# Fused attention and two feed-forward layers on one Trainium2 core: queries and keys split by pairs of heads on GpSimd and placed by DMA copies in SBUF

## The reference

```python
scores = (q @ k.T) / sqrt(D)
cum = cumsum(max(s, 0))
bias = -(cum[:, None] - cum[None, :])
scores = where(causal, -1e9, scores + minimum(bias, 0))
attn = softmax(scores)
x = attn @ v                      # then heads side by side: (2304, 512)
h = x @ w_in; solu = h * softmax(h); x = layernorm(solu) * g_ln @ w_out
out = maximum(x @ w1, x @ w2, x @ w3) @ w_out2
```

## Time and profile before

| what | value |
|---|---|
| median of 3 runs | 772.84 us (771.74 to 778.02) |
| the profiled execution's own time | 775.42 us |
| its span, first to last instruction | 773.3 us |
| mean granted TensorE clock | 0.993 |
| PE busy | 727.6 us (94%) |
| DVE busy | 418.7 us (54%) |
| ACT busy | 328.3 us (42%) |
| POOL busy | 225.7 us (29%) |

### The profile page before, as it was taken

The page is one execution under the profiler, slowest core; times in us unless marked ns, Lnnn a source line. Parts: engine busy times, 40 slices in busy tenths (PEclk is TensorE's granted clock), DMA queues, the critical chain, the costliest instruction groups (busy, mean ns, idle before and its releaser), DMA issues.

```text
span 773.3 us, 12787 instructions
## 1 busy us (share of the span) xinstructions
PE 727.6 (94%) x4312; PEld 662.6 (86%) x4312; DVE 418.7 (54%) x766; ACT 328.3 (42%) x795; POOL 225.7 (29%) x240
## 2 busy tenths in 40 slices
PE   3898999899899899999999999999999999999997
PEld 2777788788787788989898989999989999899995
DVE  8999999999985675535444364513203123032120
ACT  2888888888784443423233243412112121121111
POOL 6756669878762631404040200000000000000000
PEclk9999999999999999999999999999999999999999
DMA  6465464545341110106100031000010000100101
GB/s 154 115 165 139 135 149 119 131 124 143 88 91 43 42 37 6 41 1 176 29 0 0 0 109 56 1 21 22 1 42 1 14 28 0 41 0 0 41 0 42
DMA packets 46580, 45.28 MB, mean 59 GB/s; under 512 B 22164, under 2 KB 37652, under 8 KB 46516
## 3 DMA queue, kind: packets, MB, share of 16 engines
q1 hardware_dynamic: 46548, 44.86, 22.2%
HBM read 39.43 MB, written 5.38 MB: 58 GB/s over the span
## 4 chain that ended last, share of the span: by engine, by line
PE 66%; DMA 8%; POOL 7%; DVE 6%; issue 6%; SPq 4%; ACT 2%; POOLq 0%; ACTq 0%
PE ps L600 10%; PE ps L602 10%; PE ps L601 10%; DMA qk_raw<-in_qk_dram 8%; PE ps L532 4%; PE ps L534 4%; PE ps L533 4%; PE ps L520 4%; PE ps L522 4%; PE ps L521 4%; PE ps L613 3%; PE ps L614 3%; PE ps L615 3%; POOL qk_b L671 2%; POOL v_hl L675 2%
## 5 line engine op out<-in xcount | busy, mean ns | idle before, releaser
L602 PE MATMUL ps<-x_lo,w_hi 128*128 (+1 forms) x432 | 144.4, 334 | 0.0
L600 PE MATMUL ps<-x_hi,w_hi 128*128 128x384 f32 x432 | 144.3, 334 | 0.0
L601 PE MATMUL ps<-x_hi,w_lo 128*128 128x384 f32 x432 | 144.3, 334 | 0.0
L783 ACT ACTIVATE probs<-ps,nmax 128x576 f32<-128x576 f32 (+4 forms) x160 | 82.7, 532 | 14.2 <-DVE nmax L1002 14.2
L793 ACT ACTIVATE pt_hi<-ps 128x512 fp32r<-128x512 f32 (+1 forms) x128 | 69.7, 570 | 35.3 <-PE ps L432 32.6
L414 PE MATMUL ps<-k_a,q_a 128*128 128x288 f32 (+2 forms) x192 | 70.0, 369 | 12.9 <-DVE q_a L995 12.3
L432 PE MATMUL ps<-ident,probs 128*128 128x128 f32 x480 | 74.6, 285 | 7.7 <-DVE pt_lo L1009 3.1
L600 PEld LDWEIGHTS ps<-x_hi,w_hi 128*128 128x128 f32 x432 | 81.1, 188 | 0.2
L601 PEld LDWEIGHTS ps<-x_hi,w_lo 128*128 128x128 f32 x432 | 81.1, 188 | 0.2
L602 PEld LDWEIGHTS ps<-x_lo,w_hi 128*128 128x128 f32 x432 | 81.1, 188 | 0.0
L1009 DVE TENSOR_TENSOR pt_lo<-ps,pt_hi 128x512 fp32r<-128x512 f32 (+1 forms) x128 | 77.9, 649 | 3.4 <-ACT pt_hi L793 2.2
(11 more groups left out here) (102 smaller groups left out, 1469.1 us busy)
## 6 DMA issues: line engine op xcount, KB each, us to landing
qk_raw<-in_qk_dram SPq DMA_DIRECT2D x64, 288.0 KB, 4.3
rinvB<-rsum_dram SPq DMA_DIRECT2D x24, 192.0 KB, 4.0
stage<-in_moe_w_dram SPq DMA_DIRECT2D x18, 256.0 KB, 4.2
out_dram<-stage SPq DMA_DIRECT2D x18, 256.0 KB, 2.0
v_raw<-in_v_dram SPq DMA_DIRECT2D x32, 128.0 KB, 2.4
stage<-in_moe_w_out_dram SPq DMA_DIRECT2D x14, 256.0 KB, 2.7
stage<-in_moe_w_in_dram SPq DMA_DIRECT2D x4, 512.0 KB, 3.3
aux_dram<-setup SPq DMA_DIRECT2D x1, 576.0 KB, 4.6
```

Of the source, the lines that this page charges most:

```text
L600: pe.matmul(dst, w_hi[f][:, i, c, :], x2_hi[par][:, c, :], start=(c == 0), stop=False)
L601: pe.matmul(dst, w_lo[f][:, i, c, :], x2_hi[par][:, c, :], start=False, stop=False)
L602: mm = pe.matmul(dst, w_hi[f][:, i, c, :], x2_lo[:, c, bass.ds(g * GT, GT)], start=False, stop=(c == KC - 1))
L783: act.activation(dst, SCORES[c], ACT.Exp, bias=nmax[par][:, c:c + 1], accum_out=sums_all[:, c, bass.ds(t, 1)]).then_inc(exp_done, 1)
```

## The change

1. **Load by pairs.** A new layout `qk` holds a pair of heads on 128 partitions, k first. One DMA of 128x2x576 per pair (L286 of the changed kernel) replaces four of 64x1152. It lands in `split`, which for each of two pair buffers has four rows per partition: 0 high k, 1 high q, 2 raw k (then low k), 3 raw q (then low q).
2. **Split on GpSimd.** `scale_q` scales the raw q in place, `qk_high` writes both high parts with one instruction, `qk_low` overwrites the raw parts with the low ones. For head pair 0 these are shared out over GpSimd, ScalarE and VectorE. VectorE's `q_low` is gone from the slots; ScalarE's `split_v` goes to GpSimd too.
3. **Place by DMA.** TensorE's operands live in `oper`, one for each parity: rows `k_a`, `q_a`, `q_b`, `k_b`. Three DMAs from SBUF to SBUF per head (`copy_high`, and two in `copy_low`, each 64x2x576, 288 KB) put the halves in their places, after the head before last has its scores; the aux load follows. TensorE waits for `oper_loaded` (3 copies and aux) in place of four semaphores.
4. **First chunk on 64 partitions.** `first_of(c)` replaces the padding: chunk 0 is rows 0 to 63. The matmuls of chunk 0 have 64 stationary columns, the transposes of block column 0 have 64, `pt_high` and `pt_low` of group 0 take 448 columns instead of 512 and those of group 1 64 partitions instead of 128; `q_b` x `k_b` uses 68 partitions of 128. The memsets of the padding go.
5. **A moved wait.** TensorE waits for all of `pt_lo` of the slot before ahead of the chunk 0 scores and no longer in `turn(1)`.

```diff
+            def load_qk(pair, pb):
+                sp.dma_start(split[:, pb, 2:4, :], qkT[bass.ds(pair, 1)].rearrange("a p i s -> (a p) i s")).then_inc(qk_loaded[pb], 16)
...
+            def copy_high(h, pb):
+                rows = slice(D * h, D * (h + 1))
+                sp.dma_start(f32(oper[h][0:D, 0:2, :]), split[rows, pb, 0:2, :]).then_inc(oper_loaded[h], 16)
+
+            def copy_low(h, pb):
+                rows = slice(D * h, D * (h + 1))
+                sp.dma_start(f32(oper[h][D:P, 0:2, :]), split[rows, pb, 0:4:3, :]).then_inc(oper_loaded[h], 16)
+                sp.dma_start(f32(oper[h][0:D, 2:4, :]), split[rows, pb, 1:3, :]).then_inc(oper_loaded[h], 16)
...
             load_qk(0, 0)
+            load_qk(1, 1)
             load_v(0, 0)
-            load_qk(1, 1)
-            sp.wait_ge(rows_zeroed, 2)
+            load_v(1, 1)
+            sp.wait_ge(k0_hi_ready, 1)
+            sp.wait_ge(q0_hi_ready, 1)
+            copy_high(0, 0)
+            sp.wait_ge(k0_lo_ready, 1)
+            sp.wait_ge(q0_lo_ready, 1)
+            copy_low(0, 0)
             sp.wait_ge(cum_ready, 1)
             for h in range(2):
...
+                sp.dma_start(f32(oper[h][D:D + 4, 2:4, :]), rows).then_inc(oper_loaded[h], 16)
+            copy_high(1, 0)
+            copy_low(1, 0)
             sp.dma_start(aux_dram, setup[:, :, :]).then_inc(aux_stored, 16)
...
+            def reload_qk(pair, pb):
+                sp.wait_ge(oper_loaded[0], pair * 64 - 64)
+                sp.wait_ge(oper_loaded[1], pair * 64 - 64)
+                load_qk(pair, pb)
+
+            def refill(pair, h, pb):
+                t = 2 * pair + h
+                if h == 0:
+                    sp.wait_ge(lo_ready, pair)
+                    sp.sem_inc(sp_passed, 1)
+                sp.wait_ge(scores_done, 3 * (t - 1))
+                copy_high(h, pb)
+                copy_low(h, pb)
+                load_aux(t, h)
...
+            def reload_pair(pair, pb, known=None):
+                if known is None or known + 2 < PAIRS:
+                    reload_qk(pair + 2, pb)
+                if known == 0:
+                    sp.wait_ge(aux_stored, 16)
+                refill(pair + 1, 0, 1 - pb)
+                if known != 0:
+                    reload_v(2 * pair + 1, 1)
+                refill(pair + 1, 1, 1 - pb)
+                reload_v(2 * pair + 2, 0)
...
             def scores_4(t, par, known):
-                pe.wait_ge(q_hi_ready, t + 1)
-                pe.wait_ge(k_hi_ready, t + 1)
-                pe.wait_ge(q_lo_ready, t + 1)
-                pe.wait_ge(k_lo_ready, t + 1)
-                pe.wait_ge(aux_loaded[par], (t - par) * 8 + 16)
+                pe.wait_ge(oper_loaded[par], (t - par) * 32 + 64)
...
                     score_pass(SCORES[3], 0, 4 * P - PAD, 3, par, 3 * P - PAD)
+                    if live(known, 1) and known != 1:
+                        pe.wait_ge(pt_lo_done, 4 * (t - 1))
                     score_pass(SCORES[0], 0, P - PAD, 0, par, 0).then_inc(scores_done, 1)
...
+            def scale_q(pair, pb):
+                pool.wait_ge(qk_loaded[pb], (pair - pb) * 8 + 16)
+                q = split[:, pb, 3, :]
+                pool.tensor_scalar(q, q, SCALE, 1.0, ALU.mult, ALU.mult).then_inc(q_scaled, 1)
+
+            def qk_high(pair, pb):
+                pool.wait_ge(q_scaled, pair)
+                pool.tensor_scalar(split[:, pb, 0:2, :].bitcast(F32R), split[:, pb, 2:4, :], 1.0, 1.0, ALU.mult,
+                                   ALU.mult).then_inc(hi_ready, 1)
+
+            def qk_low(pair, pb):
+                pool.wait_ge(hi_ready, pair)
+                raw = split[:, pb, 2:4, :]
+                pool.tensor_tensor(raw.bitcast(F32R), raw, split[:, pb, 0:2, :], ALU.subtract).then_inc(lo_ready, 1)
...
+            def slot(pair, half_, pb, known):
+                t = 2 * pair + half_
                 if live(known, 1):
+                    split_v(t - 1, 1 - half_, None if known is None else known - 1)
+                if live(known, -4 + half_):
+                    if half_ == 0:
+                        scale_q(pair + 2, pb)
+                        qk_high(pair + 2, pb)
+                    else:
+                        qk_low(pair + 2, pb)
...
             def slot(t, par, known):
-                if live(known, -1):
-                    q_low(t + 1, 1 - par)
                 if live(known, 0):
```

More of the change, by code:

```diff
@@ L18, with first_of @@
 MASKED = -1.0e9
+def first_of(c):
+    return 0 if c == 0 else P * c - P // 2
 def chunk_offset(c):
-    return P * c * (c + 1) // 2
+    return sum(first_of(i + 1) for i in range(c))
 def attention_and_mlp(nc, qkT, v, s, w_in, w_out, g_ln, w1, w2, w3, w_out2, out):
-    HEADS, D, _, S = qkT.shape
+    PAIRS, _, _, S = qkT.shape
+    HEADS, D = 2 * PAIRS, P // 2
     DM, FF = w_in.shape
@@ L120, in attention_and_mlp @@
             setup = sb(a, "setup", [HEADS, 8, S])
-            qk_raw = [sb(a, f"qk_raw{i}", [P, 2, S]) for i in range(2)]
+            split_t = sb(a, "split", [P, 2, 4, ROW])
             v_raw = [sb(a, f"v_raw{i}", [P, NCH, D]) for i in range(2)]
@@ L126, in attention_and_mlp @@
             vlo_b = sb(a, "vlo_b", [D, QB])
-            q_a = [sb(a, f"q_a{i}", [P, SP], F32R) for i in range(2)]
-            qk_b = [sb(a, f"qk_b{i}", [P, SP + S], F32R) for i in range(2)]
-            k_a = [sb(a, f"k_a{i}", [P, S], F32R) for i in range(2)]
+            oper_t = [sb(a, f"oper{i}", [P, 4, ROW], F32R) for i in range(2)]
             ident_b = sb(a, "ident_b", [P, P], BF16)
@@ L136, in attention_and_mlp @@
             pt_lo = [sb(a, f"pt_lo{i}", [P, TW], F32R) for i in range(2)]
-        q_raw, k_raw = [t[:, 0, :] for t in qk_raw], [t[:, 1, :] for t in qk_raw]
-        q_b, k_b = [t[:, 0:SP] for t in qk_b], [t[:, SP:SP + S] for t in qk_b]
+        split, oper = split_t[:, :, :, 0:S], [t[:, :, 0:S] for t in oper_t]
+        k_a, q_a, q_b, k_b = [[t[:, i, :] for t in oper] for i in range(4)]
         one_rows = [setup[:, i, :] for i in (0, 2, 5, 7)]
@@ L284, in _ @@
             sp.dma_start(s_sb, s).then_inc(s_loaded, 16)
-            def load_qk(h, par):
-                rows = qkT[bass.ds(h, 1)].rearrange("a d i s -> (a d) (i s)")
-                for copy in range(2):
-                    dst = qk_raw[par][D * copy:D * (copy + 1), :, :].rearrange("p i s -> p (i s)")
-                    sp.dma_start(dst, rows).then_inc(qk_loaded[par], 16)
+            def load_qk(pair, pb):
+                sp.dma_start(split[:, pb, 2:4, :], qkT[bass.ds(pair, 1)].rearrange("a p i s -> (a p) i s")).then_inc(qk_loaded[pb], 16)
@@ new lines, in _ @@
+            reload_pair(0, 0, 0)
+            reload_pair(1, 1, 1)
+            with sp.Fori(1, 1 + KC // 2) as quad:
+                for i in range(2):
+                    pair = 2 * quad + i
+                    reload_pair(pair, i)
+                    sp.dma_start(stage[:, bass.ds(pair * FF - 2 * FF, FF)], w_in[bass.ds(pair * P - 2 * P, P), :]).then_inc(w_loaded, 16)
+            with sp.Fori(1 + KC // 2, 1 + KC // 2 + FB // 2) as quad:
+                for i in range(2):
+                    pair = 2 * quad + i
+                    reload_pair(pair, i)
+                    sp.dma_start(stage[:, bass.ds(pair * DM + KC * FF - (2 + KC) * DM, DM)],
+                                 w_out[bass.ds(pair * P - (2 + KC) * P, P), :]).then_inc(w_loaded, 16)
@@ L676, in split_v @@
                                    ALU.subtract).then_inc(v_lo_ready, 1)
-            qk_high(0, 0, 0)
-            k_low(0, 0)
+            k0_hi, k0 = split[:, 0, 0, :], split[:, 0, 2, :]
+            pool.wait_ge(qk_loaded[0], 16)
+            pool.tensor_scalar(k0_hi.bitcast(F32R), k0, 1.0, 1.0, ALU.mult, ALU.mult).then_inc(k0_hi_ready, 1)
+            pool.wait_ge(k0_hi_ready, 1)
+            pool.tensor_tensor(k0.bitcast(F32R), k0, k0_hi, ALU.subtract).then_inc(k0_lo_ready, 1)
+            scale_q(1, 1)
+            qk_high(1, 1)
+            qk_low(1, 1)
             pool.wait_ge(setup_pool, 5)
+            pool.wait_ge(setup_dve, 1)
             def split_win(piece):
@@ L728, in normalize @@
                 pool.tensor_scalar(ln[i][:, :], ln[i][:, :], st[:, 3:4], st[:, 6:7], ALU.add, ALU.mult).then_inc(ln_done, 1)
-            slot(HEADS - 2, 0, HEADS - 2)
-            slot(HEADS - 1, 1, HEADS - 1)
+            for t in range(HEADS - 4, HEADS):
+                slot(t // 2, t % 2, t // 2 % 2, t)
             pool.wait_ge(xa_done, HB)
@@ L873, in lnT_high @@
                     act.activation(lnT_hi[:, f, :], ps[:, 4 + f % 4, 0:GT], ACT.Copy).then_inc(lnT_hi_done, 1)
-            act.wait_ge(q_lo_ready, HEADS)
-            act.wait_ge(k_lo_ready, HEADS)
+            for i in range(2):
+                act.wait_ge(oper_loaded[i], 64 * PAIRS)
             x_high(0, 0, 0, True)
@@ L974, in _ @@
             for i in range(2):
[L975 to L977 removed]
+                dve.memset(v_raw[i][P - PAD:P, 0, :], 0.0)
+            dve.memset(sums_all[:, :, :], 0.0)
```

(4 more changed lines are left out.)

211 lines of the change are left out of this document (83 added, 128 removed).

## The result

The changed kernel takes **832.0 us** (822.85 to 837.05, 4 runs) against 773.19 us before (4 runs beside it): ratio 1.071, 95% interval 1.062 to 1.080. The forecast was 766.4 us, its range 758 to 786. The profiled execution has a span of 827.4 us, 54.1 more than before.

The account below looks back on a forecast made before the run. In attention VectorE was taken as the fuller engine, with `q_low` lengthening slots. 24 slots gave -8.2 us, the last four -2.5, the start +4.3: -6.4, so 772.84 to 766.4 us; range 758 to 786.

Parts of the forecast that it names:

- 28s - 187.0: Whole kernel's change in us for a slot (one head's turn in attention) of s: 24 slots, last four and start.
- s = 6.45: Attention slot without `q_low` on VectorE: 2.68 us until the values start, plus 3.77 of exponential tail; 6.79 before.
- 28.1 for the last four: Last four attention slots: 4 x 6.45 + 2.3 us for sums and inversion, 30.64 before, a gain of 2.5.
- start term: First score, waiting for head pair 0's split and copies: 16.6 us, +4.3 us, bounds +2 and +7.
- chunk 0 without padding: Attention's first chunk: 448 columns for 512 save 64 ns off the path; shorter weight loads may give 0.05 to 0.1.
- not above 6.79 by this term alone, since nothing in the loop gets longer: Upper bound on the attention slot from taking `q_low` off VectorE; the lower bound was TensorE's own work, 6.19 us.
- x = 1.2: DMA time in us of one 288 KB SBUF copy, between the loads' 0.98 and the store's 1.4; copies just hide.
- my own formula: DMA time for a pair of slots, 5.0 + 6x us: other traffic plus six copies of x us each.
- rival A: Copies bound the attention slots at x = 1.4: 6.7 us a slot, +0.6 us, 773.4; chance 0.17.
- B: Copies bound slots hard, x = 1.6: 7.3 us a slot, +17.4, 790 us, TensorE waiting before `scores_4`; chance 0.20.
- the deadline: An odd head's copies, issued 2.5 us into slot t-2 and needed 8.4 us later, were said to fit.
- GpSimd's 2.85 us a head: GpSimd's split work per head, replacing 2.81 to 3.8 us and working a pair ahead; costed at nothing.

Follow-up runs that it names:

- experiment 6: Changed kernel with copies reading and writing alternate partitions and chunk 0's transposes and value matmuls back on 128 rows: 766.4 us, 0.989.
- experiment 2: Changed kernel, but from head 2 on each copy moves only 288 of 576 columns (scores of stale data): 783.6 us, 1.014.
- 5: Changed kernel with copies on alternate partitions: only reading side 877.5 us, only written side 796.3, both sides 781.3 (slots of 6.94).
- experiment 1: Changed kernel, but SyncE issues an even head's copies ahead of the load of the pair after next: 823.5 us, 1.066.
- experiment 3: Changed kernel with transposes and value matmuls of chunk 0 and block column 0 back on 128 partitions: 807.6 us, 1.044.
- 7: The kernel of experiment 6 with only the values' matmuls of key block 0 back on 64 rows: 772.8 us, 0.999.
- 8: ScalarE's exponential of chunk 0 moved ahead of `pt_high` 2 and 3: on experiment 6 760.3 us, 0.986; on the kernel before 772.4, 0.998.

## Why the prediction was wrong

- **The sum's structure held, once both faults were taken away.** 28s - 187.0 with s = 6.45 and 28.1 for the last four describes experiment 6: 6.49 a slot, 27.8, 766.4 us. Its start term does not: head 3 is 1.5 us late there and not 4.3. That the time meets the forecast to the tenth is luck; that the slot meets it by both of its parts is not. The step by which VectorE is no longer full and the two row maxima come next was right in that kernel.
- **Failed: "chunk 0 without padding", costed at a gain of 0.05 to 0.1 us.** It costs 0.46 us a slot (6.95 in experiment 2 and 6.94 in 5, 6.49 in 6), 28 x 0.46 = 13 us. I counted columns and weight loads, which do get shorter, and not what happens between neighbours of different row counts. The bound "not above 6.79 by this term alone, since nothing in the loop gets longer" was no bound: it was argued, and no row stood behind it.
- **Failed: x = 1.2**, "halfway between the two near rows". It is 1.48 by my own formula, above the store's 1.4. The row nearest in kind, partitions of one half, was the store's; the loads' 300 GB/s alternated between halves, which I wrote down and then averaged in. At 1.48 the queue needs 13.9 us a pair, which is over the 1.39 from which the kernel turns slower and between rival A's 1.4 and B's 1.6. The place was the one that B named, TensorE's wait before `scores_4`.
- **Failed: the deadline.** "3.6 us of data and 1.8 fixed fit, and for an even head the pair's load may lie ahead, 7.2" leaves out the `w_in` piece: 512 + 576 KB at 223 GB/s are 5.0 us ahead of 3 x 1.48 and 1.8 fixed, 11.2 us in all, against 8.4. A mean over pairs (the 5.0) holds no deadline; the worst pair does, and it returns every four heads.
- **Failed: the price of a late copy.** B was costed as a longer slot, 28 x 7.3 - 187.0 = +17.4. Formula and x = 1.48 would give 6.95 a slot, +7.6 us. The waits of 1.8 to 4.1 us brought 7 to 24 us at 1.2 GHz each. That lost 27 us in all, twice the waits' own 14, a term that no rival had. The trace of before had one such case: TensorE's wait of 2.3 us for `pt_lo`, which the prediction read in the earlier trace rows, ended at 211.68, and from 213.3 to 216.7 the granted clock was 0.50. The clock of 1.00 in the earlier trace rows hid it, and I did not look.
- **The start**: first score at 17.12 for 16.6 forecast, +4.8 for +4.3. VectorE's part took 1.69 for my 2.4, and the landing 4.5 from the aux DMAs' issue at 12.62, which stand behind the copies. (The 1.17 of the loop was not free of GpSimd's work either: `q_low` took from 0.76 to 2.46 us in the kernel before. So 2.46 against 1.17 does not measure what the two engines do to each other.) But head 3 is 11.3 us late. The other 6.5 are copies that are late from head 1 on (waits of 0.42 and 1.27 us) and a slower TensorE. The clock column shows 1.00 there, but the first matmul of 288 columns takes 0.61 us at 31.14 and 0.59 at 40.38 and only at 48.11 the 0.38 that it takes at the upper level; in the kernel before it took 0.37 at 23.84. The shares of the two are not separated. In experiment 6, where the first score comes at 15.55, head 3 is 1.5 us late (36.35).
- **Costed at nothing, and rightly**: `split_v` off ScalarE, GpSimd's 2.85 us a head and the moved wait show up in no wait of TensorE in the changed kernel. GpSimd's waits for loads grew to 85.8 us, for which "no longer waits for a load for long" was wrong, at no cost there; in experiment 1 they did reach TensorE, through the split of v that stands behind them.

**What is shown and what is argued.** Shown by taking it away: the copies' bytes (2), their partitions (5), the 64 rows (3, 6, 7), the tail (8). Read from rows alone: the lower clock's 27 of the 45 us, since no run had late copies at a full clock, and the part of the `w_in` piece in the missed deadlines. Not explained: the slow run with only the source spread, and why longer waits brought less of the lower clock in experiment 3.
